# Expert results scattered to the tokens' own rows, and read back in token order by plain loads

## The reference

```python
# q, k, v: (2, 8, 768, 64); 4 sink positions, window 128
scores = q @ k.T / sqrt(64), kept where key < 4 or 0 <= query - key < 128
x = softmax(scores) @ v                       # -> x: (1536, 512), one row per token

do_compute = x @ w_skip > 0                   # the other tokens pass through unchanged
e = argmax(x @ w_gate); gate = softmax(x @ w_gate)[e]       # 8 experts
x[do_compute] += gate * (relu(x @ w1[e]) @ w2[e])           # w1: 512x1024, w2: 1024x512

h = x @ w_in                                  # 512x2048
g = (a0 + a1 h + a2 h^2 + a3 h^3) / (1 + |b0||h| + |b1| h^2 + 1e-6)
out = g @ w_out                               # 2048x512
```

## Time and profile before

| | us |
|---|---|
| time, median of 3 runs | 667.9 (667.66 to 668.02) |
| span of the profiled execution | 665.0 |
| time less span | 2.9 |
| TensorE matmul busy | 572.1 (86%) |
| VectorE busy | 494.8 (74%) |
| GpSimd busy | 338.6 (51%) |
| ScalarE busy | 335.1 (50%) |
| mean granted TensorE clock | 0.951 of full |

### The profile page before, as it was taken

The page is one execution under the profiler, slowest core; times in us unless marked ns, Lnnn a source line. Parts: engine busy times, 40 slices in busy tenths (PEclk is TensorE's granted clock), DMA queues, the critical chain, the costliest instruction groups (busy, mean ns, idle before and its releaser), DMA issues. The chain is left out here.

```text
span 665.0 us, 9671 instructions
## 1 busy us (share of the span) xinstructions
PE 572.1 (86%) x3152; PEld 480.0 (72%) x3153; DVE 494.8 (74%) x471; ACT 335.1 (50%) x663; POOL 338.6 (51%) x245
## 2 busy tenths in 40 slices
PE   5678688798967999999687897989699999899985
PEld 5667577686957999999575675666588866688763
DVE  2698898974261426445239999899998999999994
ACT  2555546454601333345055575665756656755662
POOL 3453443400012664553126887668677666677763
PEclk9589989799977999999889999999899999999998
DMA  8773729800962859996122112100201000100001
GB/s 166 157 154 79 160 42 255 335 0 1 372 245 81 306 204 352 398 402 267 47 96 64 32 48 63 33 32 17 80 1 32 1 0 1 63 1 0 1 0 63
DMA packets 37782, 77.33 MB, mean 116 GB/s; under 512 B 3120, under 2 KB 14384, under 8 KB 37744
## 3 DMA queue, kind: packets, MB, share of 16 engines
q1 hardware_dynamic: 33616, 64.79, 31.5%
q0 software_dynamic: 2832, 9.70, 4.5%
q10 hardware_dynamic: 1296, 2.36, 0.9%
HBM read 63.21 MB, written 13.63 MB: 116 GB/s over the span
## 5 line engine op out<-in xcount | busy, mean ns | idle before, releaser
L1361 DVE RECIPROCAL den<-den 128x512 f32<-128x512 f32 x48 | 160.3, 3341 | 5.1 <-POOL den L1151 5.1
L1210 PE MATMUL moe_h_ps<-x_hi,work 128*128 128x512 f32 x384 | 101.4, 407 | 11.3 <-ACT line L1291 10.8
L1210 PEld LDWEIGHTS moe_h_ps<-x_hi,work 128*128 128x128 f32 x384 | 71.0, 190 | 37.4 <-ACT line L1291 20.2
L1229 PE MATMUL o_ps<-w_out_hi,g_hi 128*128 128x512 f32 x192 | 80.3, 418 | 19.8 <-ACT g_hi L1308 11.5
L1144 POOL TENSOR_TENSOR g_lo<-g,g_hi 128x512 fp32r<-128x512 f32 x48 | 62.0, 1291 | 63.2 <-ACT g_hi L1308 63.1
L1308 ACT ACTIVATE g_hi<-g 128x512 fp32r<-128x512 f32 x48 | 30.3, 632 | 117.2 <-DVE g L1367 117.2
L1151 POOL TENSOR_TENSOR den<-den,side 128x512 f32<-128x512 f32 x48 | 61.9, 1289 | 35.5 <-ACT den L1282 35.3
L1153 POOL TENSOR_TENSOR g<-g,square 128x512 f32<-128x512 f32 x48 | 77.9, 1623 | 1.0 <-ACT g L1287 0.8
L1230 PE MATMUL o_ps<-w_out_lo,g_hi 128*128 128x512 f32 x192 | 76.5, 398 | 0.0
L1367 DVE TENSOR_TENSOR g<-g,den 128x512 f32<-128x512 f32 x48 | 69.1, 1439 | 5.0
L863 PEld LDWEIGHTS h_ps<-xT,w_sb 128*128 128x128 f32 x576 | 67.6, 197 | 2.0 <-issue 1.4
(11 more groups left out here) (163 smaller groups left out, 1076.0 us busy)
## 6 DMA issues: line engine op xcount, KB each, us to landing
w_raw<-in_w SPq DMA_DIRECT2D x32, 512.0 KB, 6.6
w_sb<-in_w SPq DMA_DIRECT2D x8, 2048.0 KB, 11.2
k_raw<-in_k SPq DMA_DIRECT2D x16, 384.0 KB, 7.3
q_raw<-in_q SPq DMA_DIRECT2D x16, 384.0 KB, 10.1
rows_dram<-zero_rows SPq DMA_DIRECT2D x1, 4864.0 KB, 19.0
w_in_raw<-in_w_in POOLq DMA_DIRECT2D x8, 512.0 KB, 6.1
w_out_raw<-in_w_out SPq DMA_DIRECT2D x16, 256.0 KB, 2.6
v_sb<-in_v SPq DMA_DIRECT2D x4, 768.0 KB
```

Of the source, the lines that this page charges most:

```text
L1210: mm = pe.matmul(h_ps[c % 2][:], w[:, k, f], x[:, k, :], start=n == 0 and k == 0, stop=n == len(parts) - 1 and k == z.KD - 1)
L1229: pe.matmul(o_ps[i][:], g_hi[c % 2][:, tok(i)], w_hi[:, c, :], start=c == 0, stop=False)
L1361: nc.vector.reciprocal(den[d][:], den[d][:]).then_inc(inv_ready, 1)
```

## The change

Rows of tokens are stored twice after attention, to `rows_dram` (from which the experts gather) and to `mixed_dram`. The result of an expert tile is scattered by an indirect DMA of GpSimd over the tokens' own rows in `mixed_dram`, and the last stage reads `mixed_dram` in token order with plain loads. The slot area, its zeros, `keep.row`, `idle`, `own` and `place` go. Token numbers are carried with 2048 subtracted, so that an empty slot (a sum of 0) becomes 2048: `slot_home` keeps it, out of bounds, and its row isn't written; `slot_token` is capped to 1535, a row that exists. The diff, cut:

```diff
             # attention, SyncE
-            sp.dma_start(rows_dram[z.N:, :].rearrange("(t p) d -> p t d", p=P),
-                         zero[:].unsqueeze(1).to_broadcast([P, z.SLOT_TILES, z.D])).then_inc(zero_stored, 16)
-            sp.wait_ge(zero_stored, 16)
...
             with sp.Fori(0, z.B) as b:
                 sp.wait_ge(normed, done(b, STEPS - 1))
-                sp.dma_start(rows_dram[bass.ds(b * z.S, z.S), :].rearrange("(t p) d -> p t d", p=P),
-                             keep.x_tok[:, bass.ds(b * z.QT, z.QT), :]).then_inc(keep.rows_stored, 16)
+                for rows in (rows_dram, mixed_dram):
+                    sp.dma_start(rows[bass.ds(b * z.S, z.S), :].rearrange("(t p) d -> p t d", p=P),
+                                 keep.x_tok[:, bass.ds(b * z.QT, z.QT), :]).then_inc(keep.rows_stored, 16)
             # attention, GpSimd
-            pool.memset(zero[:], 0.0).then_inc(zeroed, 1)
             # routing, VectorE (token_id now starts at -2048)
-            nc.vector.tensor_copy(keep.slot_token[:], slots_ps[:, 0, 0:z.SLOT_TILES]).then_inc(tokens_ready, 1)
+            nc.vector.tensor_scalar(keep.slot_token[:], slots_ps[:, 0, 0:z.SLOT_TILES], float(z.NOWHERE), float(z.N - 1), ALU.add, ALU.min).then_inc(tokens_ready, 1)
+            nc.vector.tensor_scalar(keep.slot_home[:], slots_ps[:, 0, 0:z.SLOT_TILES], float(z.NOWHERE), None, ALU.add).then_inc(tokens_ready, 1)
...
-            step(nc.vector.tensor_scalar(idle[:], active[:], -1.0, 1.0, ALU.mult, ALU.add))
-            step(nc.vector.tensor_tensor(slot_b[:], idle[:], token_id[:], ALU.mult))
-            step(nc.vector.scalar_tensor_tensor(out=own[:], in0=active[:], scalar=float(z.N), in1=slot_b[:], op0=ALU.mult, op1=ALU.add))
-            step(nc.vector.tensor_tensor(keep.row[:], slot_a[:], own[:], ALU.add))
             # experts, SyncE
-            sp.sem_inc(y_stored, 32)
+            sp.sem_inc(y_free, 2)
             # experts, ScalarE: store() and its calls go
-                with act.If(t > 0):
-                    store(t - 1)
...
             # experts, VectorE, ahead of y
-                dve.wait_ge(y_stored, 16 + t * 16)
+                dve.wait_ge(y_free, t + 1)
             # experts, GpSimd
+            def scatter(t):
+                with pool.If(n > t):
+                    pool.wait_ge(y_ready, 1 + t + 1)
+                    if t > 0:
+                        pool.wait_ge(y_stored, t * 16)
+                        pool.sem_inc(y_free, 1)
+                    pool.indirect_dma_start(mixed_dram, bass.IndirectOffsetOnAxis(ap=keep.slot_home[:, t:t + 1], axis=0), y_sb[:, t % 2, :], None,
+                                            bounds_check=z.N - 1, oob_is_err=False).then_inc(y_stored, 16)
...
             for t in range(1, z.SLOT_TILES):
                 gather(t)
+                if t >= XS_RING - 1:
+                    scatter(t - (XS_RING - 1))
                 if t >= XS_RING - 1 and t - (XS_RING - 1) < 2 * z.KD:
                     split_w_in(t - (XS_RING - 1))
+            for t in range(z.SLOT_TILES - (XS_RING - 1), z.SLOT_TILES):
+                scatter(t)
             pool.wait_ge(halves, 4 * z.KD)
-            pool.wait_ge(y_stored, 32 + n * 16)
+            with pool.If(n > 0):
+                pool.wait_ge(y_stored, n * 16)
             # rational, SyncE, ahead of coef and w_out
+            for i in range(MT):
+                sp.dma_start(first_tile(i), mixed_dram[i * P:(i + 1) * P, :]).then_inc(first_loaded[i], 16)
             # rational, GpSimd
-            def find(m):
-                pool.tensor_copy(place[:], keep.row[:, bass.ds(m * MT, MT)]).then_inc(placed, 1)
-                pool.wait_ge(placed, m)
-            def gather(m, i):
+            def load(m, i):
                 pool.wait_ge(x2T_done, m * MT + i - 1)
-                pool.indirect_dma_start(x2[:, i % 2, :], None, rows_dram, bass.IndirectOffsetOnAxis(ap=place[:, i:i + 1], axis=0),
-                                        bounds_check=rows_dram.shape[0] - 1, oob_is_err=False).then_inc(rows_gathered[i % 2], 16)
+                pool.dma_start(x2[:, i % 2, :], mixed_dram[bass.ds((m * MT + i) * P, P), :]).then_inc(rows_loaded[i % 2], 16)
...
-            for i in range(MT):
-                pool.indirect_dma_start(first_tile(i), None, rows_dram, bass.IndirectOffsetOnAxis(ap=keep.row[:, i:i + 1], axis=0),
-                                        bounds_check=rows_dram.shape[0] - 1, oob_is_err=False).then_inc(first_gathered[i], 16)
```

More of the change, by code:

```diff
@@ L40, in __init__, with attention @@
         self.EXPERT_TILES = self.N // P
-        self.ROWS = self.N + self.SLOTS
-def attention(nc, z, keep, q, k, v, w_route, rows_dram, n_sink, window):
+        self.NOWHERE = 2 ** 11
+        assert self.N <= self.NOWHERE
+def attention(nc, z, keep, q, k, v, w_route, rows_dram, mixed_dram, n_sink, window):
     G = z.H // 2
@@ L483, in routing @@
         token_id = sb("token_id", [P, T])
-        idle = sb("idle", [P, T])
-        own = sb("own", [P, T])
         one_e = sb("one_e", [P, E])
@@ L729, in split_w2_low, with experts @@
         nc.vector.tensor_tensor(keep.w2_lo[:, f, :], keep.w2_raw[:, f, :], keep.w2_hi[:, f, :].bitcast(F32), ALU.subtract).then_inc(keep.w2_lo_ready, 1)
-def experts(nc, z, keep, w1, w2, rows_dram, w_in):
+def experts(nc, z, keep, w1, w2, rows_dram, mixed_dram, w_in):
     with ExitStack() as ctx:
@@ L906, in body @@
                     act.activation(xT[:], xT_ps[:], ACT.Copy).then_inc(xT_ready, 1)
-                with act.If(t > 0):
-                    store(t - 1)
-            def store(t):
-                t = tile(t)
-                act.wait_ge(y_ready, 1 + t + 1)
-                act.wait_ge(y_stored, 32 + t * 16)
-                act.dma_start(rows_dram[bass.ds(z.N + t * P, P), :], y_sb[:, bass.ds(t % 2, 1), :].rearrange("p o d -> p (o d)")).then_inc(y_stored, 16)
-            n = tiles(act, first, start, body, nothing)
-            with act.If(n > 0):
-                store(n - 1)
+            tiles(act, first, start, body, nothing)
         @block.vector
@@ L1380, in program @@
         keep.ident = sb("ident", [P, P])
-        keep.row = sb("row", [P, z.TT], U32)
         keep.n_tiles = sb("n_tiles", [P, z.E], I32)
@@ L1402, in program @@
             keep.rows_stored = ctx.enter_context(nc.semaphore("own_rows_stored"))
[L1403 removed]
+            attention(nc, z, keep, q, k, v, w_route, rows_dram, mixed_dram, n_sink, window)
             keep.w1_sb = [own(f"w1_sb{i}", [P, z.KD, z.F]) for i in range(2)]
@@ L1409, in program @@
             routing(nc, z, keep, w1, w2, rows_dram)
-            experts(nc, z, keep, w1, w2, rows_dram, w_in)
-        rational(nc, z, keep, rows_dram, w_out, coef, out)
+            experts(nc, z, keep, w1, w2, rows_dram, mixed_dram, w_in)
+        rational(nc, z, keep, mixed_dram, w_out, coef, out)
 def kernel(q, k, v, n_sink, window, moe_w_skip, moe_w_gate, moe_w1, moe_w2, moe2_w_in, moe2_w_out, moe2_a, moe2_b):
```

35 lines of the change are left out of this document (15 added, 20 removed).

## The result

The kernel after the change takes 672.51 us (median of 11 runs, 669.0 to 677.24) against 667.66 us for the kernel before on the same chip (11 runs, 666.54 to 669.83). The ratio is 1.0071, 95% interval 1.0048 to 1.0095: slower by about 4.8 us. Forecast were 672.2 us and a range of 666.5 to 678.5. The sum came out. Of its five terms the first two did (0, and the seam to routing, whose size varies between profiles); the other three were mis-sized, two of them by more than the whole sum.

The account below looks back on a forecast made before the run. Bounds: ScalarE and DMA in routing, TensorE in the expert and last stages, late DMAs at seams. 3.7 + 4.0 - 0.8 - 2.6 = +4.3 on 665.0, plus 2.9 for the median, gives 672.2 us; range 666.5 to 678.5.

Parts of the forecast that it names:

- Term 1: Attention: dropping the store of 4864 KB of zeros counts for nothing, with bounds of 0.5 us either way.
- Term 2: Seam to routing: an extra 1.57 MB store ahead of w2 on SyncE's queue delays it, +3.7 us (+0.5 to +4.7).
- Term 3: Experts: scatters in GpSimd's order delay the w_in splits and the stage's end, +4.0 us (+0.4 to +9).
- rival B: Experts: GpSimd falls behind by 6 us and more, +9 instead of +4, 677.2 us; chance 0.14.
- slowly behind: Experts: GpSimd's round of 13.5 to 14.5 us slowly loses ground to the y's, 13.06 us each.
- later splits leave the crowded time of the weight loads: Experts: argument against a larger GpSimd lag; the last split should wait less for w_in, minus 2 to 3 us.
- TensorE doesn't notice: Experts: late gathers are taken up by VectorE's idle 4.7 us ahead of each y, so TensorE isn't delayed.
- The part on time: End of experts: with GpSimd on time, last scatter issued at 325.5 and landed at 328.8, +1.7 us.
- Rival C: End of experts: 17 skipped gather and scatter blocks behind the last scatter cost perhaps 3 us, 675.2 us; chance 0.10.
- Term 4: Start of last stage: plain loads replace four gathers and remove TensorE's wait, -0.8 us (0 to -1.0).
- what is late next is the warm-up itself: Start of last stage: rows land inside TensorE's warm-up, so all of the 1.04 us wait goes and no more.
- Term 5: Inside last stage: plain loads replace GpSimd's index copy, wait and indirect DMAs, -2.6 us (0 to -3.6).

Follow-up runs that it names:

- e8: Changed kernel with the 4.98 MB store of zeros and its wait put back in attention; 671.21 us, ratio 1.0044 to the kernel before.
- e7: Kernel before with a second x_tok store of the same size in the same place, to rows nobody reads; 670.86 us, ratio 1.0009.
- e2: Changed kernel with the second batch entry's mixed_dram store issued behind the first w2 pieces and both w1 loads; 669.76 us, ratio 1.0023.
- e1: Changed kernel with each split of w_in put ahead of the scatter in GpSimd's loop; 666.31 us, ratio 0.9972 to the kernel before.
- e3: Changed kernel with the 3 KB coef_sb load ahead of the four row loads of the last stage; 671.42 us, ratio 1.0047.
- e5: Changed kernel with GpSimd's copy, wait and indirect row loads restored for the last stage's later rounds; 680.88 us, ratio 1.0177.
- e6: Changed kernel with GpSimd's copy of four columns and its wait restored at c = 0, row loads kept plain; 672.84 us, ratio 1.0080.
- e9: Changed kernel with the next piece of w_in asked for before the present one is split; 680.21 us, ratio 1.0168 to the kernel before.
- e12: Changed kernel without the gather and scatter blocks that these inputs skip (tiles 9 to 18); 672.70 us, ratio 1.0057.
- e10: Changed kernel with splits ahead of scatters, second mixed_dram store later, coef_sb first and w_in pieces asked for one step ahead; 663.10 us, ratio 0.9909.
- e11: Changed kernel with splits first, later mixed_dram store, coef_sb first, w_in prefetched except pieces 6 and 7, asked for just before splitting; 659.51 us, ratio 0.9856.

## Why the prediction was right, and where only its sum was

**Term 1, attention, 0.** Right: e8 puts the zeros back and the store is issued at the same time.

**Term 2, the seam to routing, +3.7.** Right in place: e7 makes it alone, and e2 takes it away (first split at 9.6 us again). The size fits this pair of profiles: y(0) moved by 3.8 us, 0.3 of it ahead of routing, and in e7 it is 4.3 from the store to y(0). But over the eight profiles in which both stores stand ahead of w2 (the kernel after, e1, e3, e5, e6, e8, e9, e12) the stretch from store to y(0) is 1.8 to 4.0 us longer than the 54.5 us of the kernel before, 2.9 in the mean, and e2 gave 2.8 us by the medians. 3.7 lies inside that range, above its middle.

**Term 3, the experts, +4.0: mis-sized, 8.9 measured** (0.5 from y(0) to y(8), 8.4 from there to the last stage). The step that failed is the sum of GpSimd's chain. It had 105.5 us between the first and the last scatter (108.0, less 2 to 3); the profile has 111.0 (225.26 to 336.30). The waits for w_in were 43.7 us and not 39.8; the subtractions 20.6, not 19.1; five gathers 7.4, not 5.5 (two take 1.95 and 1.99 us); the gaps 2.8, not 3.9. The last scatter should have come at 331 (327 and the 3.8 us of the seam) and came at 336.3. So the lag of 6 us and more that rival B named, and its price for this term (+9), are what happened, with 0.14 against the forecast's 0.59; its reasons, gaps of 0.7 us or scatters of 1.5, are not (the scatters took 1.05).

Nor did GpSimd fall "slowly behind": it kept pace for three rounds, lost 9 us in the next three and made up 3 in the last two. That "later splits leave the crowded time of the weight loads" held for the last two only, with waits of 4.5 and 3.8 us; the three before them, 7.1, 6.6 and 8.0, were longer than the mean of 5.3 that the sum had used.

"TensorE doesn't notice" held in this profile but for one late gather (301.97), and fails in others: y(0) to y(8) is 104.3 to 108.4 us in seven profiles with the same order of gather, scatter and split (after, e2, e3, e5, e6, e8, e12). The two longest, e8 and e12, are splits that met VectorE's w_lo, as in e9. That may be why the times of the kernel after spread wider (669.0 to 677.2); no run shows it. The part on time was sized well: where GpSimd keeps pace (e10, e11) the last stage starts 7.1 us after y(8), +2.1 over the kernel before; +1.7 was written. A scatter in a quiet time (the last one) lands 2.7 us after its issue, nearer to the 2.6 us worked out from the Trainium skill's "DMA: Bandwidth & Descriptors", section "Anatomy of one DMA", than to the gather's 3.3 us that I took.

**Rival C, the skipped blocks.** Refuted by e12 (5.32 against 5.31 us from the last scatter to the last stage). The Trainium skill's "Advanced Engine Details and Errata", section "Control Flow Timing", gives a compare-and-branch about 108 ns, from which the prediction estimated 1.8 us for all 17, less than the 2.7 us of the scatter's landing. The trace agrees that they are hidden; their own time it doesn't show.

**Term 4, start of the last stage, -0.8: the reason was wrong, and -0.2 is measured** (-0.2 to -1.2 over the eight profiles named at e3, so the size was within what these profiles show). The step "what is late next is the warm-up itself" failed. The first rows did come in time, but coef_sb, moved behind 1 MB, was late next, 5.2 us from issue to landing. I named it as the bound and didn't work it out. The small sum hides three parts: the pause of 1.04 us goes, the transposes take some 1.5 us less at the higher granted clock, and the wait of 2.68 us comes. With coef_sb first (e3) the stretch is 2.5 us shorter than in the kernel before.

**Term 5, inside the last stage, -2.6, "3.6 at most": wrong, -7.2.** The cap added the times freed on GpSimd. e6 gives back the copy (0.18) and a wait (0.30) and the stretch doesn't change; e5 gives back 1.1 us more at c = 0 and 0.5 for each other DMA, and loses 7.4 us. What VectorE loses isn't what GpSimd needs more: where the two start together it loses the rest of GpSimd's chain, 4.37 us for an add of 0.86. The Trainium skill's "SBUF — State Buffer", section "SBUF: two separate sides", says that the pair of ports that the two engines share is an exclusive lock held for a whole instruction by whichever starts first. The trace agrees for one instruction: in the ordinary case VectorE's add ends 0.5 to 0.6 us after the GpSimd operation that it met. It shows more in the rare case, the whole chains above. The rows I had would have warned me: at c = 0 the multiply of the earlier trace rows had 3.22 - 1.59 = 1.6 us to give, and the add 4.32 less what an add takes elsewhere, both more than the 1.4 us that I let c = 0 give.

**The sum.** 3.8 + 8.9 - 0.2 - 7.2, and 0.5 at the end (the granted clock is 0.50 in the last matmuls' 3 us, 663.5 to 666.5, where it was 1.00 from 658 to 661 before, and one takes 0.63 us for 0.40), is 5.8, against 4.3 forecast. The last 0.5 is the difference from the last reciprocal to the end of the span, and the clock is a reason for it that no run tests. Two errors of 4.9 and 4.6 us with opposite signs cancel. (The medians are 4.8 us apart, the two profiled executions 5.8.) That the median met 672.2 us is largely luck: the reasons were right for terms 1 and 2 and the direction of the others, and the sizes of terms 3 and 5 were each wrong by more than the whole forecast sum.

## What to carry to other kernels

- Before moving an operation that waits into an in-order engine, sum the chain behind it with its waits as they are, and give the sum's error its full weight: what the chain is behind is paid at the barrier. Here three rounds out of eight, with the longest waits for a DMA, made all of it. Putting the wait behind the independent work (e1) gave 5.6 us at this barrier for a swap of two calls.
- A small edit on GpSimd can cost or give several times its own length on VectorE, in either direction: look for an operation of VectorE that starts within 0.1 us of a chain of GpSimd's without gaps, and for what waits behind it. Removing waits isn't a gain in itself (e9: 15.4 us more from y(0) to y(8), and 680.21 us for 672.51), and putting two back was one (e11: -3.6 us).
- One profile of a kernel is one draw. Between profiles of kernels that agree in a stretch, y(0) to y(8) varied by 4 us and the store to y(0) by 2 us: a term of that size needs the same mark in several profiles.
- A load of a few KB that the next stage needs first goes ahead of the large ones on its queue.

## What the runs showed of the hardware that I had not expected

- A waiting operation of VectorE usually has its turn behind one operation of GpSimd, even in a chain without gaps (45 of 45 times in the last stage of the kernel after: the add of chunk 0 at 0.86 with GpSimd's neighbour at 1.74). Where both start within about 0.1 us of each other it waited for the whole chain (before and e5, three times each: that add at 4.32 and 4.37 with GpSimd's at 1.28).
- Beside GpSimd's split of w_in, two operations of VectorE on 128x1024 take 4.56 us, undisturbed 2.35 (e9, e11), and GpSimd's own subtraction 3.25 in place of 2.38.
- Issuing an indirect DMA takes GpSimd 1.0 to 1.1 us in a quiet time and up to 2.0 beside VectorE's subtractions (1.99 at 278.80 in the kernel after, with w_lo from 278.54); a plain one 0.6.
- 3 KB behind four loads of 256 KB take 5.2 us to land; ahead of them they take 3.0 (e3).
